# Chunk products regrouped, early weight splits moved, a flag read sooner: gated linear attention feeding two feed-forward stages on one Trainium2 core

## The reference, cut to what matters

```python
# attention: 4 x 8 heads, 768 positions, head size 48
f = 1 / (1 + exp(-f_logit))
for t in range(S):
    state = f[t][:, None] * state + outer(k[t], v[t])
    y[t] = q[t] @ state
x = y as (3072 tokens, 384)
# first feed-forward: 384 -> 1536 -> 384
x = ((x @ w_a) * (x @ w_b)) @ w_out
# second: 4 experts, 384 -> 1024 -> 384, all of them on every token
p = domain_probs / (domain_probs.sum(-1) + 1e-9)
out = sum_e p[:, e] * (relu(x @ w1[e]) @ w2[e])
```

## Time and profile before

| | |
|---|---|
| median of 3 runs | 1440.24 us (1439.63 to 1440.3) |
| the profiled execution | 1440.07 us |
| its span, first to last instruction | 1438.3 us |
| PE busy | 1411.0 us (98%) |
| PE weight loads busy | 1287.7 us (90%) |
| DVE, ACT, POOL busy | 481.8, 392.3, 287.5 us |
| chain that ended last | PE 96%, issue 1%, POOL 1%, DVE 1% |
| mean granted TensorE clock | 0.98 of full speed |

### The profile page before, as it was taken

How to read it: one execution, slowest core, us unless ns; L and a number is a source line. 1 busy time by engine, 2 the same in 40 slices (tenths; PEclk the granted TensorE clock), 3 DMA queues, 4 the chain that set the end, 5 groups by cost and what they waited for, 6 DMA issues and landing times.

```text
span 1438.3 us, 19724 instructions
## 1 busy us (share of the span) xinstructions
PE 1411.0 (98%) x7897; PEld 1287.7 (90%) x7897; DVE 481.8 (33%) x922; ACT 392.3 (27%) x739; POOL 287.5 (20%) x225
## 2 busy tenths in 40 slices
PE   4999999999999999999999999999999999999999
PEld 3788988988989999989999999999999999999998
DVE  6776555545532222212222222222222222222222
ACT  4444343333323222232111221111321112211111
POOL 6453121211201100024111331111511112211110
PEclk6599999999999999999999999999999999999999
DMA  7443222222200000002000110000200000000001
GB/s 157 118 124 96 59 62 45 60 63 44 49 13 12 12 1 1 1 24 66 1 0 1 33 56 0 1 1 1 77 12 0 1 0 23 23 23 22 23 23 44
DMA packets 43694, 49.35 MB, mean 34 GB/s; under 512 B 4688, under 2 KB 42064, under 8 KB 43600
## 3 DMA queue, kind: packets, MB, share of 16 engines
q1 hardware_dynamic: 43600, 48.04, 13.0%
HBM read 38.58 MB, written 4.72 MB: 30 GB/s over the span
## 4 chain that ended last, share of the span: by engine, by line
PE 96%; issue 1%; POOL 1%; DVE 1%; DMA 0%; ACT 0%; DVEq 0%; POOLq 0%; SPq 0%
PE bank L1000 20%; PE bank L1001 20%; PE bank L1002 20%; PE bank L1130 9%; PE bank L1129 9%; PE bank L1128 9%; PE bank L995 3%; PE bank L990 2%; PE bank L967 2%; PE bank L976 1%; PE bank L952 1%; DMA raw<-wa 0%; POOL wab_lo L673 0%; DVE unit L743 0%; POOL unit L657 0%
## 5 line engine op out<-in xcount | busy, mean ns | idle before, releaser
L935 DVE SCALAR_TENSOR_TENSOR h_lo<-bank,h_hi 128x512 fp32r<-128x512 f32 x192 | 132.8, 692 | 600.9 <-ACT h_hi L638 600.9
L638 ACT ACTIVATE h_hi<-bank 128x512 fp32r<-128x512 f32 x192 | 115.0, 599 | 628.6 <-PE bank L1002 628.6
L1130 PE MATMUL bank<-slot_hi,h_lo 128*128 128x384 f32 x768 | 258.5, 337 | 0.0
L1128 PE MATMUL bank<-slot_hi,h_hi 128*128 128x384 f32 x768 | 258.1, 336 | 0.0
L1129 PE MATMUL bank<-slot_lo,h_hi 128*128 128x384 f32 x768 | 258.0, 336 | 0.0
L1000 PE MATMUL bank<-xs_hi,slot_hi 128*128 128x512 f32 x576 | 225.4, 391 | 3.0 <-issue 3.0
L1001 PE MATMUL bank<-xs_hi,slot_lo 128*128 128x512 f32 x576 | 226.2, 393 | 0.0
L1002 PE MATMUL bank<-xs_lo,slot_hi 128*128 128x512 f32 x576 | 226.0, 392 | 0.0
L1000 PE MATMUL bank<-xs_hi,wab_hi 128*128 128x384 f32 x576 | 199.5, 346 | 0.0
L683 POOL TENSOR_TENSOR xs_lo<-xt,xs_hi 128x512 fp32r<-128x512 f32 x72 | 91.1, 1293 | 523.6 <-ACT xs_hi L562 523.6
L1001 PE MATMUL bank<-xs_hi,wab_lo 128*128 128x384 f32 x576 | 194.3, 337 | 0.0
(11 more groups left out here) (84 smaller groups left out, 1548.2 us busy)
## 6 DMA issues: line engine op xcount, KB each, us to landing
unit<-fkq SPq DMA_DIRECT2D x62, 216.0 KB, 4.2
raw<-w SPq DMA_DIRECT2D x64, 192.0 KB, 2.6
v_in<-v_chunks SPq DMA_DIRECT2D x32, 144.0 KB, 3.9
out<-ostage SPq DMA_DIRECT2D x24, 192.0 KB, 1.9
xt<-ystage SPq DMA_DIRECT2D x48, 72.0 KB, 2.2
raw<-wa SPq DMA_DIRECT2D x6, 384.0 KB, 4.7
raw<-wb SPq DMA_DIRECT2D x6, 384.0 KB, 3.1
raw<-wo SPq DMA_DIRECT2D x6, 384.0 KB, 3.7
```

Source lines behind the costliest of these rows:

```text
L638: eng.activation(h_hi[:, j % 2, :], ps_up[j % 4][:, :], ACT.Relu).then_inc(s_hhi, 1)
L935: eng.scalar_tensor_tensor(out=h_lo[:, j % 2, :], in0=ps_up[j % 4][:, :], scalar=0.0, in1=h_hi[:, j % 2, :].bitcast(f32), op0=ALU.max, op1 ...
L1128: eng.matmul(o, hh, w_hi, start=(f == 0), stop=False)
L1130: mm = eng.matmul(o, hl, w_hi, start=False, stop=(f == FT2 - 1))
```

## The change

Three edits. In `output(u)` all state products stand first, the first of them alone clearing the bank's accumulation (`start`), and the six value products follow. The first seven weight pieces go to slots -16, -15, -13, -12, -10, -9 and -7, behind `gates` of the units of those slots, with the loads that follow on them. The flag is loaded to a register at slot `STRONG_AT` = 167 on each engine, only the branch stays at the loop's end, and a wait for it in `up_2` goes.

```diff
+    STRONG_AT = CMIN_AT + 9
@@ split_at
         if r < R0:
-            return J[0] - 6 + 2 * r
+            return J[0] + 2 + r // 2 * APART + r % 2
@@
-        def general_form(eng):
+        def is_strong(eng):
             eng.wait_ge(s_min, 5)
-            return eng.If(eng.value_load(strong[0:1, 0:1], min_val=0, max_val=1))
+            return eng.value_load(strong[0:1, 0:1], min_val=0, max_val=1)
@@ on each engine
             for j in range(BEGIN, 3 * N1):
+                if j == STRONG_AT:
+                    flag = is_strong(eng)
...
-            with general_form(eng):
+            with eng.If(flag):
@@ output(u)
+                with_state = range(1 - half_of(u), CPU)
+                for cc in with_state:
+                    t = slice(cc * CH, (cc + 1) * CH)
+                    eng.matmul(o[0:P2, t], st_before(u, cc)[0:P2, :], unit_ring[ring(u)][0:P2, Q, t],
+                               start=(cc == with_state[0]), stop=False, skip_group_check=True)
                 for cc in range(CPU):
                     t = slice(cc * CH, (cc + 1) * CH)
-                    begins = half_of(u) == 0 and cc == 0
-                    if not begins:
-                        eng.matmul(o[0:P2, t], st_before(u, cc)[0:P2, :], unit_ring[ring(u)][0:P2, Q, t], start=True,
-                                   stop=False, skip_group_check=True)
                     for n, start in enumerate((0, 64)):
                         a = (n * CPU + cc) * CH
                         vv = (cc * 2 + n) * D
                         mm = eng.matmul(o[start:start + D, t], v_in[:, u % VRING, vv:vv + D],
-                                        att[two(u)][:, a:a + CH], start=begins, stop=True, skip_group_check=True)
+                                        att[two(u)][:, a:a + CH], start=False, stop=True, skip_group_check=True)
@@ up_2
                     eng.wait_ge(s_h, N1)
-                    eng.wait_ge(s_min, 5)
```

## The result

The changed kernel takes 1415.14 us (median of 4 runs, 1413.62 to 1415.16), the kernel before 1440.27 in the same comparison: a ratio of 0.9823, 95% interval 0.9806 to 0.984. The profiled execution went from 1440.07 to 1415.16 us, 24.9 less (span 1438.3 to 1413.4). 27.0 were forecast.

What follows compares the result with a forecast made beforehand. PE was taken as the bound, with 96% of the chain of waits and never without work from about 67 us on. Output 15.2, start 10.8 and flag 1.0 sum to 27.0 us off 1440.07: 1413 us, range 1406 to 1423.

Steps and rivals of the forecast that it cites:

- The output: Outputs of units 5 to 31 at full clock: 0.57 us saved per first half, 0.56 per second, 15.2 us in all.
- the passes: Six value passes in a unit's output: 0.87 us, taken from the scores; 0.96 and 0.80 were weighed too.
- Rival (c): Output: regrouping does nothing, only start and flag gain, without the 3.3 us; 1431.6 us, chance 0.07.
- Rival (d): Output: a slower kernel, each value pass in a row waiting for its weight loads; chance 0.03.
- The splits and the start: Start: first feed-forward product 10.4 - 2.9 + 3.3 = 10.8 us earlier, at 56 us in place of 66.89.
- the five early outputs: Start: regrouped outputs of five units at low clock save 0 to 3.5 us, 3.3 taken.
- the clock I leave as it is: PE's clock at the start: expected unchanged, 0.50 through the small products and some 3 us into the dense ones.
- scans of 3 us and more: DVE at the start: sign that the forecast is wrong, if scans last so long through the steps of units 1 to 4.
- some 3 us: First dense products: time they run at clock 0.50 before the clock reaches 1.00, as before the change.
- The flag: Hole ahead of the second feed-forward stage: 1.2 us gained less 0.2 at slot 167, net 1.0 (-1.5 to 3.0).
- Rival (a): Start: splits collide with scans and gates, first product only about 3 us sooner; 1421 us, chance 0.17.
- rival (b): Start: clock up early or PE not the bound at low clock, full 15.9 us gained, value passes at 0.11; 1406 us, chance 0.07.

Runs made afterwards that it cites:

- e4_output_late: Kernel before with only the new output order, and that for units 5 to 31 alone; 1422.47 us, ratio 0.9872.
- e9_alternate: Changed kernel with state and value products of second-half units alternating again, in another order with chunks shifted; 1424.44 us, ratio 0.9888 against the kernel before.
- e2_splits: Kernel before with only the new slots of the first weight splits; 1432.51 us, ratio 0.9943.
- e5_dve_lo: Changed kernel with the low parts of the first seven weight pieces subtracted on DVE in place of POOL; 1411.57 us, ratio 0.9805 against the kernel before.
- e6_xk: Changed kernel with the first up-projection waiting for each slice of its block apart; 1411.12 us, ratio 0.9797 against the kernel before.
- e7_fill: Changed kernel with seven idle products on PE ahead of the second stage's branch; 1414.38 us, ratio 0.9823 against the kernel before.
- e8_dve_xk_fill: Changed kernel with DVE's low parts, slices waited for apart and seven idle products ahead of the branch; 1408.86 us, ratio 0.9784 against the kernel before.
- e1_output: Kernel before with only the new order of the output, in all units; 1419.74 us, ratio 0.9857.

## Why the prediction came out right, step by step

**The output (15.2 forecast, 17.5 measured).** The sum over a unit was 0.17 + 0.22 + 0.32 + the six passes, and that is what the rows show: 0.17 + 0.22 + 0.32 + 0.79 = 1.50. The one mis-sized term is the passes: 0.87 was taken from the scores, 0.79 was measured, next to the other value weighed there, 0.80. The scores were the only row with six passes in a run, but they are another product with other shapes, and the pace within a pair told more. 0.08 us in each of 27 units, 0.09 in the second halves, is the 2.3 us. Rival (c), that regrouping does nothing, fell with e4_output_late and e9_alternate. Rival (d), a slower kernel because each pass in a row would wait for its weight loads, fell too: the twelve loads of six passes come to 12 x 0.122 = 1.46 us of load time, and the six passes take 0.79 us, though all of them use the same 128 rows.

**The splits and the start (10.8 forecast, 9.05 measured).** `kv` of unit 0 came at 18.34, not 19.6, 11.6 us earlier and not 10.4: the chain behind the gates is 1.2 us shorter than allowed. The five unit steps behind it gained 12.1 - 11.6 = 0.5 us, where 3.3 - 2.9 = 0.4 was forecast. That is near by luck: with the splits alone (e2_splits) these steps took 3.8 us more, not 2.9, and the new order with its higher clock then gave back 4.3 and not 3.3 (from `kv` of unit 0 to `kv` of unit 5: 35.8 us before, 39.6 in e2_splits, 35.3 in the changed kernel). The 3.3 us that the forecast took for the five early outputs at the low clock no run shows. At clock 0.50 the output of unit 3 takes 2.57 us up to `kv` of unit 4 (47.30 to 49.87) where it took 3.19 (55.15 to 58.34), 0.62 less; unit 4's ran at 1.00 already. The last step failed: the forecast let the first product come as PE comes to it, at 56. It was late by 3.1 us. Before, the block was ready 66.89 - 66.22 = 0.67 us ahead of PE, but with PE at the pace of before; "the clock I leave as it is" was the false premise under it. In the regrouped order the clock rises in the units at the start, PE's part of the steps of units 4 and 5 shrinks (8.55 to 4.6 us), and the way over the transfer and the split of the block doesn't (7.76 and 7.75). So 12.1 became 9.05. e2_splits shows it from the other side: at 0.50 throughout there is no hole. That the splits would stretch the scans was named with a sign ("scans of 3 us and more"), which was a poor sign, since the kernel before had such scans too (3.57 to 4.15 us). It came true in three steps with 3.39, 5.43 and 5.63 us. The version that takes the subtractions off POOL, e5_dve_lo, is 3.6 us faster, scans and clock together.

**The clock behind the start (nothing forecast, 1.4 lost).** The clock falls in the same hole of 3.38 us, so the dense products run at 0.50 for 5.8 us and not 2.9; the forecast had "some 3 us". Where the hole is shorter (e5_dve_lo, e6_xk) they begin at full clock, though in e6_xk it falls 2.3 us later. The loss is that of one execution: in e7_fill, with the same start, it was 3.4 us at 0.50.

**The flag (1.0 forecast; 1.07 gained in the hole, 1.3 lost behind it in the profiled execution).** The value taken, 1.2 less 0.2, held: without the load at the branch 1.07 us of the 2.99 are gone and 1.92 stay. At slot 167, where the load now stands, the trace shows no wait of PE: from 300 us to the hole it has only the 0.33 us for `h_lo` at 604.91, which stood there before too. What in the 1.92 us is the branch, and what a fetch of code, no run parts: the profile's instruction queues moved two packets within the hole of before (631.82 to 634.81) and one within that of the changed kernel (606.71 to 608.63). The fall of the clock was not foreseen, and it isn't a matter of the hole's length alone: it stayed up behind 2.99 us and fell behind 1.92. What decides it is open.

**The sum.** 27.0 + 2.3 (passes) + 1.3 (unit 0 and steps) - 3.1 (the block) + 0.1 (the flag) - 2.7 (the clock, twice) = 24.9. The forecast was near because errors of both signs met. Rival (a), most of the early gain given back, has its mechanism in part (the moved splits cost 3.8 us by themselves), but 9.05 us remained, not 3. Of rival (b) the premise came true, the clock came up early, and its conclusion did not: the start was no longer bound by PE.

## What to carry to other kernels

Group small products by how they tile the array: each trip from full-array products into tiles and back cost 0.33 us, as much as three value passes. Before counting a saving of one engine as a saving of the start, compare each transfer and each split on the way with the new pace of that engine, its clock included: slack measured at the low clock can be gone when the clock rises (here 0.67 us of it became a wait of 3.38 us). And look at the clock behind each hole that remains: where it fell, that cost 1.3 and 1.4 us beside the hole itself. Waiting for slices in place of a block brought the first product 2.75 us forward. Idle products in a hole cost no more than 0.3 us here (2.25 us from the last down-projection product to the next stage in the changed kernel, 2.28 in e7_fill, 2.56 in e8_dve_xk_fill) and the clock stayed up behind them, but the medians show no gain clear of their spread.

## What the runs showed of the hardware that was not expected

- PE's clock rose before the first dense product in all eight kernels whose units 0 to 3 have their six value passes in a row, and in none of the four with the alternating order there. By stretch it was 0.74 to 0.90 in e1_output and 0.50 in the same stretches of e2_splits, in two of which PE was busy 7.00 of 7.00 us. When and how often it rose differed: three times in the changed kernel, twice in e7_fill with the same start, once in e8_dve_xk_fill. What sets the moment is open.
- Column-tiled passes with 48-column weights follow one another at some 0.12 us ((0.79 - 0.21) / 5), with two weight loads of 0.12 us in each, so 1.46 us of loads in passes of 0.79 us.
- Three scans on DVE took 5.43 us next to four POOL instructions in a row (24.25 to 29.97 us), and 1.04 us without them; with the subtractions of weights on DVE itself (e5_dve_lo) the kernel was 3.6 us faster than with them on POOL.
- Keeping a flag in a register took 1.07 us out of the hole at a branch, and 1.92 us stayed (over all traces 2.89 to 3.26 us with the load at the branch, 1.83 to 2.44 without).
